# The last stage's first product as Strassen's seven block products, and its second product in a pass of its own

## What is computed

```python
def _moe2_ref(x, w_in, w_out, alpha):          # x: 4608 x 512, w_in: 512 x 2048, w_out: 2048 x 512
    h = x @ w_in
    g = np.maximum(h, 0.0) + alpha * np.minimum(h, 0.0)
    return g @ w_out
```

## Time and profile before

| | |
|---|---|
| time, median of 3 | 1443.22 us (1442.37 to 1443.36) |
| the profiled execution's own time | 1444.12 us |
| its span | 1442.4 us |
| mean granted clock of TensorE | 0.983 |
| busy: PE, DVE, ACT, POOL | 95%, 46%, 28%, 13% |
| chain that ended last, by engine | PE 86%, DVE 5%, ACT 3%, DMA 2% |
| last stage, first matmul to the end of the span | 676.7 to 1442.4 us |

### The profile page before, as it was taken

One profiled execution on the slowest core, in us unless ns is written; L12 is line 12 of the kernel. 1 busy time (PEld: TensorE's weight loads), 2 busy tenths in 40 slices (PEclk: granted clock), 3 DMA queues, 4 the chain that ended last, 5 costly groups with the idle time before them and its releaser, 6 DMA issues.

```text
span 1442.4 us, 18986 instructions
## 1 busy us (share of the span) xinstructions
PE 1366.5 (95%) x6741; PEld 1119.5 (78%) x6742; DVE 659.0 (46%) x949; ACT 398.8 (28%) x632; POOL 189.2 (13%) x234
## 2 busy tenths in 40 slices
PE   4998589999979999996999999999999999999998
PEld 3877468888868888885787878878788787887887
DVE  3677652222545525435545344453544435444343
ACT  5888231112333313223212121121211212112121
POOL 4564121111212212221000000000000000000000
PEclk9999799999989999998999999999999999999999
DMA  7785252111444314133201010010100101001000
GB/s 268 263 272 182 74 192 85 44 44 44 155 141 163 132 71 160 56 141 109 74 0 58 0 49 9 0 58 0 55 3 0 58 0 58 0 4 55 0 30 15
DMA packets 71483, 112.58 MB, mean 78 GB/s; under 512 B 6816, under 2 KB 38560, under 8 KB 70816
## 3 DMA queue, kind: packets, MB, share of 16 engines
q1 hardware_dynamic: 64192, 91.79, 18.8%
q0 software_dynamic: 6112, 19.93, 4.0%
q10 hardware_dynamic: 1152, 0.52, 0.2%
HBM read 84.17 MB, written 27.53 MB: 77 GB/s over the span
## 4 chain that ended last, share of the span: by engine, by line
PE 86%; DVE 5%; ACT 3%; DMA 2%; issue 2%; SPq 2%; DVEq 0%; ACTq 0%; POOL 0%; POOLq 0%
PE ps L320 9%; PE ps L322 9%; PE ps L321 9%; PE ps_o L322 7%; PE ps_o L320 7%; PE ps_o L321 7%; PE ps_y L322 5%; PE ps_y L320 5%; PE ps_h L320 5%; PE ps_y L321 5%; PE ps_h L322 5%; PE ps_h L321 5%; PE ps_hT L1248 2%; SPq L434 2%; PE ps_sr L1139 1%
## 5 line engine op out<-in xcount | busy, mean ns | idle before, releaser
L762 ACT ACTIVATE gT_hi<-act_g 128x512 fp32r<-128x512 f32 (+1 forms) x144 | 87.7, 609 | 563.2 <-DVE act_g L1054 563.2
L1051 DVE TENSOR_SCALAR neg<-ps,alpha 128x512 f32<-128x512 f32 (+1 forms) x144 | 103.7, 720 | 291.1 <-PE ps L322 291.1
L320 PE MATMUL ps<-yT_hi,w_hi 128*128 128x512 f32 (+1 forms) x576 | 221.9, 385 | 5.7 <-DVE yT_lo L1041 5.7
L322 PE MATMUL ps<-yT_hi,w_lo 128*128 128x512 f32 (+1 forms) x576 | 221.0, 384 | 0.0
L321 PE MATMUL ps<-yT_lo,w_hi 128*128 128x512 f32 (+1 forms) x576 | 221.0, 384 | 0.0
L320 PE MATMUL ps_o<-w_hi,gT_hi 128*128 128x512 f32 x544 | 212.0, 390 | 0.9 <-DVE w_lo L793 0.9
L322 PE MATMUL ps_o<-w_hi,gT_lo 128*128 128x512 f32 x544 | 212.2, 390 | 0.0
L321 PE MATMUL ps_o<-w_lo,gT_hi 128*128 128x512 f32 x544 | 211.8, 389 | 0.0
L1057 DVE TENSOR_TENSOR gT_lo<-act_g,gT_hi 128x512 fp32r<-128x512 f32 (+1 forms) x144 | 95.4, 663 | 97.2 <-ACT gT_hi L762 97.2
L320 PEld LDWEIGHTS ps<-yT_hi,w_hi 128*128 128x128 f32 x576 | 108.5, 188 | 32.4 <-DVE yT_lo L1041 9.3
L320 PE MATMUL ps_h<-w_hi,xgT_hi 128*128 128x512 f32 x296 | 122.1, 412 | 9.6 <-DVE w_lo L793 7.7
(11 more groups left out here) (190 smaller groups left out, 1738.0 us busy)
## 6 DMA issues: line engine op xcount, KB each, us to landing
stage<-in_moe_w SPq DMA_DIRECT2D x32, 1024.0 KB
xs_all<-in_xT SPq DMA_DIRECT2D x8, 1024.0 KB, 6.3
xN_all<-in_xN SPq DMA_DIRECT2D x8, 1024.0 KB, 6.2
rows_x<-xrow SPq DMA_DIRECT2D x32, 256.0 KB, 2.5
yg<-rows_y SPq DMA_DIRECT2D x128, 64.0 KB, 1.9
out_rows<-orow SPq DMA_DIRECT2D x32, 256.0 KB, 2.1
stage<-in_moe_w_in SPq DMA_DIRECT2D x4, 1024.0 KB
stage<-in_moe_w_out SPq DMA_DIRECT2D x4, 1024.0 KB
```

The costliest lines, as they stand in the source:

```text
L320: pe.matmul(out, s_hi, m_hi, start=start, stop=False)
L322: return pe.matmul(out, s_lo, m_hi, start=False, stop=stop)
L762: act.activation(gT_hi[:, c % 2, f, 0:w], act_g[:, 0:w], ACT.Copy).then_inc(g_hi_ready, 1)
L1051: dve.tensor_scalar(neg[:, 0:w], ps_1[f][:, 0:w], 0.0, alpha[:, ft:ft + 1], ALU.min, ALU.mult)\
```

## The change

The first product of a batch of 544 rows (512 tokens and 32 state rows, which were a ninth group before) is now Strassen's scheme in Winograd's form. The batch's transposed rows are cut in four blocks (two halves of the 512 inputs by two halves of 272 rows), w_in in four (inputs by features); seven products P1 to P7 of sums of such blocks, each 2x3 matmuls of 272 columns for each of 8 tiles c of 128 features (`product`), take the place of eight. Four sums of w_in's blocks are made on DVE during experts 0, 2, 4 and 6, a quarter of the columns each, from an extra load, stored in memory (`sums_w`), and loaded back; seven chunks of 1 MB follow expert 7 in place of four (`block_of`). Four sums of the rows' blocks are made on DVE, and seven high and seven low parts in place of four, the low ones between c=7's additions. The seven products of a c lie in seven PSUM banks; one ACT copy and seven DVE additions (`add`) put the four quarters of the features together in `gb`, and SP stores them, not rectified, to `acts` in memory. PE waits before each product until the addition that frees its bank is done.

The second product runs after all first products, tile by tile (`down`): SP loads a tile's 16x128 features for 128 rows (1 MB in 512-byte rows; the two tiles of state rows in 128-byte pieces), DVE rectifies in two operations over 2048 elements, ACT and DVE split, PE takes 48 matmuls of 512 columns. Buffers are double. w_out is loaded over `stage` early in the first pass and split during the last batch, in w_in's freed places. At the stage's start the rows of batch 0 are fetched by SP and ACT in half each, and ACT rounds and DVE rests three more weight chunks ahead of them.

The core of the diff:

```diff
-FC = 2
-NC_ = KFF // FC
+NP = KFF // 2
+FH = FF // 2
+TB = S + NS
+TH = TB // 2
+P1, P2, P6, P7, P4, P5, P3 = range(7)
+SLOT = (0, 1, 4, 2, 3, 5, 6)
...
+        tT = yz_[:].rearrange("p (m k t) -> p m k t", m=4, k=2)
+        b_of = (yT[:, 0:2, 0:TH], yT[:, 2:4, 0:TH], tT[:, 1], tT[:, 2], tT[:, 3], tT[:, 0], yT[:, 2:4, TH:TB])
...
+            with sp.Fori(1, E // 2) as pair:
+                load_raw(pair - 1)
+                for par in range(2):
+                    e = 2 * pair + par
+                    for i in range(CH):
+                        load_weights(e * CH + i, i, expert_chunk(e, i), (e - 1) * CH + i + 1)
+                    if par == 0:
+                        store_sums(pair - 1)
+            load_raw(3)
+            block_of = (WI[:, 0:2, 0:FH], WI[:, 2:4, 0:FH], sums_w[2], WI[:, 2:4, FH:FF], sums_w[1], sums_w[0], sums_w[3])
+            for i in range(7):
+                if i == 2:
+                    store_sums(3)
+                load_weights(E * CH + i, i % CH, block_of[i], (E - 1) * CH + i + 1)
...
+            def load_acts(t, g, k, again):
+
+                if again:
+                    wait_apart(sp, g_lo_ready, t - 1)
+                sp.dma_start(gt[k % 2][:], acts[bass.ds(g, 1)].rearrange("a p f t -> (a p) f t")[:, :, k * P:(k + 1) * P])\
+                  .then_inc(g_loaded[k % 2], 16)
+
+            def load_states(t, k):
+                wait_apart(sp, g_lo_ready, t - 1)
+                for j in range(4):
+                    sp.dma_start(gt[k][:, :, j * NS:(j + 1) * NS], acts[4 * k + j][:, :, S:TB]).then_inc(g_loaded[k], 16)
...
+            with sp.Fori(0, B - 1) as g:
+                wait_apart(sp, b_lo_ready, 7 * g + 7)
+                for c in range(NP):
+                    if c < QB:
+                        load_y(g + 1, (c,))
+                    store_acts(g, c)
...
+            for c in range(NP):
+                store_acts(B - 1, c)
+            for par in range(2):
+                for h in range(2):
+                    sp.wait_ge(acts_stored[h][par], 16 * (1 + B * NP // 2))
+            sp.wait_ge(product_ready[P3], B * NP)
+            load_acts(1, 0, 1, False)
...
+                    t = 4 * g + k
+                    load_acts(t + 2, g if k < 2 else g + 1, (k + 2) % 4, True)
+                    store_tile(t, k, [g * TB + k * P])
+            for k in range(4):
+                t = XT - 4 + k
+                if k < 2:
+                    load_acts(t + 2, B - 1, k + 2, True)
+                else:
+                    load_states(t + 2, k - 2)
+                store_tile(t, k, [(B - 1) * TB + k * P])
...
+            round_chunk((E + 1) * CH, 0, 0, 1)
...
+            for i in range(1, 3):
+                round_chunk((E + 1) * CH + i, i, i, 1)
...
+            def copy_p1(g, c):
+
+                n = NP * g + c
+                act.wait_ge(product_ready[P1], n + 1)
+                if not (isinstance(n, int) and n == 0):
+                    act.wait_ge(u2_ready, n)
+                act.activation(part[0][:], ps_p[P1][:, 0:TH], ACT.Copy).then_inc(p1_copied, 1)
...
+            def tile_high(t, k):
+                act.wait_ge(g_ready, t + 1)
+                if not (isinstance(t, int) and t < 2):
+                    act.wait_ge(o_ready, t - 1)
+                act.activation(g_hi[k % 2][:], gt[k % 2][:], ACT.Copy).then_inc(g_hi_ready, 1)
...
+                        dve.wait_ge(raw_loaded, 64 * pair + 64)
+                        dve.tensor_tensor(sum_w[:, 0], raw_w[:, 2], raw_w[:, 3], ALU.add).then_inc(s1_made, 1)
+                        dve.tensor_tensor(sum_w[:, 2], raw_w[:, 0], raw_w[:, 2], ALU.subtract)
+                        dve.wait_ge(s1_made, pair + 1)
+                        dve.tensor_tensor(sum_w[:, 1], sum_w[:, 0], raw_w[:, 0], ALU.subtract).then_inc(s2_made, 1)
+                        dve.wait_ge(s2_made, pair + 1)
+                        dve.tensor_tensor(sum_w[:, 3], raw_w[:, 1], sum_w[:, 1], ALU.subtract).then_inc(sums_made, 1)
...
+            for i in range(3):
+                rest_chunk((E + 1) * CH + i, i, i, 1)
...
+            def sums_12(g):
+                dve.wait_ge(yT_ready, 2 * g + 2)
+                dve.tensor_tensor(tT[:, 0], b12, b11, ALU.subtract).then_inc(t_ready, 1)
+                dve.wait_ge(t_ready, 4 * g + 1)
+                dve.tensor_tensor(tT[:, 1], b22, tT[:, 0], ALU.subtract).then_inc(t_ready, 1)
+
+            def sums_34(g):
+                dve.tensor_tensor(tT[:, 2], b22, b12, ALU.subtract).then_inc(t_ready, 1)
+                dve.wait_ge(t_ready, 4 * g + 2)
+                dve.tensor_tensor(tT[:, 3], b21, tT[:, 1], ALU.subtract).then_inc(t_ready, 1)
...
+                    n, par = NP * g + c, c % 2
+                    again = not (isinstance(n, int) and n == 0)
+                    ahead = c == NP - 1 and not last
+                    dve.wait_ge(p1_copied, n + 1)
+                    free_acts(dve, 0, NP // 2 * g + c // 2, par)
+                    add(gb[par][:, 0, 0:TH], P2, n, part[0][:], c11_ready)
+                    if again:
+                        dve.wait_ge(u5_ready, n)
+                    add(part[1][:], P6, n, part[0][:], u2_ready)
+                    if ahead:
+                        low(g + 1, P1)
+                    dve.wait_ge(u2_ready, n + 1)
+                    if again:
+                        dve.wait_ge(c22_ready, n)
+                    add(part[2][:], P7, n, part[1][:], u3_ready)
+                    if ahead:
+                        low(g + 1, P2)
+                    dve.wait_ge(u3_ready, n + 1)
+                    free_acts(dve, 1, NP // 2 * g + c // 2, par)
+                    add(gb[par][:, 1, 0:TH], P4, n, part[2][:], c21_ready)
+                    if ahead:
+                        low(g + 1, P6)
+                    add(gb[par][:, 1, TH:TB], P5, n, part[2][:], c22_ready)
+                    if ahead:
+                        low(g + 1, P7)
+                        low(g + 1, P4)
+                    add(gb[par][:, 0, TH:TB], P5, n, part[1][:], u5_ready)
+                    if ahead:
+                        low(g + 1, P5)
+                        low(g + 1, P3)
+                    dve.wait_ge(u5_ready, n + 1)
+                    add(gb[par][:, 0, TH:TB], P3, n, gb[par][:, 0, TH:TB], c12_ready)
+                    if not last:
+                        if c == 4:
+                            turn_y(g + 1, 0, 9)
+                        if c == 5:
+                            turn_y(g + 1, 9, 17)
+                            sums_12(g + 1)
+                        if c == 6:
+                            sums_34(g + 1)
+                    else:
+                        for i, f in enumerate((c, NP + c)):
+                            dve.wait_ge(wo_hi_ready, 2 * c + i + 1)
+                            dve.wait_ge(product_ready[P4], n + 1)
+                            dve.tensor_tensor(w_out(w_lo, f), raw_out(f), w_out(w_hi, f).bitcast(F32), ALU.subtract)                               .then_inc(wo_lo_ready, 1)
+                        if c == 5:
+                            rectify(0, 0, 1)
+                        if c == 6:
+                            tile_low(0, 0)
...
+            free = {P1: p1_copied, P2: c11_ready, P6: u2_ready, P7: u3_ready, P4: c21_ready, P5: u5_ready, P3: c12_ready}
+
+            def product(p, g, c):
+
+                n = NP * g + c
+                if c == 0:
+                    pe.wait_ge(b_lo_ready, 7 * g + p + 1)
+                if isinstance(n, int) and n == 0:
+                    pe.wait_ge(w_lo_ready, E * CH + SLOT[p] + 1)
+                else:
+                    pe.wait_ge(free[p], n)
+                for k in range(2):
+                    mm = three(pe, ps_p[p][:, 0:TH], w_in(w_hi, p, k, c), w_in(w_lo, p, k, c),
+                               b_hi[p][:, k, :], b_lo[p][:, k, :], k == 0, k == 1)
+                mm.then_inc(product_ready[p], 1)
+
+            def group(g):
+                for c in range(NP):
+                    for p in range(7):
+                        product(p, g, c)
...
+            def down(t, k, fresh=False):
+                pe.wait_ge(g_lo_ready, t + 1)
+                pe.wait_ge(o_copied, t + 1)
+                for i in range(KFF):
+                    f = i // 2 + i % 2 * NP
+                    if fresh:
+                        pe.wait_ge(wo_lo_ready, i + 1)
+                    mm = three(pe, ps_o[k % 2][:], g_hi[k % 2][:, f, :], g_lo[k % 2][:, f, :], w_out(w_hi, f), w_out(w_lo, f),
+                               i == 0, i == KFF - 1)
+                mm.then_inc(o_ready, 1)
 
             pe.wait_ge(w_lo_ready, CH * (E + 1))
             pe.wait_ge(yT_ready, 1)
             for _ in range(11):
                 pe.matmul(ps_o[0][:], w_hi[0][:, 0:P], w_hi[0][:, 0:DM], start=True, stop=True)
-            with pe.Fori(0, B - 1) as g:
-                group(g, 4)
-            group(B - 1, 4)
-            group(B, 2)
+            group(0)
+            with pe.Fori(1, B) as g:
```

(25 more changed lines are left out.)

349 lines of the change are left out of this document (185 added, 164 removed).

## The result

The changed kernel takes 1427.31 us (median of 4 runs, 1426.94 to 1427.9), the kernel before 1442.86 beside it: ratio 0.9893, 95% interval 0.9875 to 0.991. It is 15.6 us faster, where 11.8 were forecast; 1431.4 was the forecast, 1416 to 1452 the range.

The account below looks back on a forecast made before the run. The last stage was taken as bound by TensorE's matmul columns. 338.7 + 1.6 + 2 + 15.2 + 369.5 + 5 = 732.0 against 760.9 us, with +17.1 at the start: -11.8, so 1431.4 us, range 1416 to 1452.

Parts of the forecast that it names:

- First product: First pass of the last stage: 2688 matmuls of 272 columns at 0.126 us, 338.7 us, a gain of 41.3 us.
- rival d: First product: weight load not hidden at the short width, 0.188 us a matmul, +166 us, 1598; chance 0.02.
- rival (c): First product's short matmuls run at the second product's pace per column, 0.1203 us: -15 us, 1416; chance 0.05.
- Second pass: Second product in its own pass: the same 1632 matmuls at 0.2264 us, 369.5 us, with loads hidden.
- The start: Start of last stage: seven weight blocks in place of four move first product from 676.70 to 693.8, +17.1 us.
- half clock: PE's slow stretch after waiting: 1.6 us charged at the first products, and 1.6 us again after the gap between passes.
- Hand-overs: Batch to batch in the first pass: no stall by a hair, 0.3 us charged for each of 7, 2 us.
- Rival (a): VectorE bounds the hand-overs at c=7 of each batch: 2.9 us each, +18 us, 1450; chance 0.12.
- State tiles: Last two tiles of the second pass, loaded in 128-byte pieces: 5 us of stall.
- rival b: State tiles' loads cost by packet count instead of bytes: +15 us, 1446; chance 0.13.
- Between the passes: Waits of 2.6 us before tile 0 and 11.1 before tile 1, then half clock 1.6: 15.2 us (12 to 20).

Follow-up runs that it names:

- the run with extra work: Changed kernel plus four more unread VectorE subtractions of 224 elements in each of seven batch hand-overs, ahead of P3's last addition: 1434.73 us.
- moved weights: Changed kernel with only allocation order changed, w_hi0 and w_lo0 at 116,128 to 181,664 instead of 17,088 to 82,624: 1415.63 us, ratio 0.9815.

## Why the prediction was right, and where its terms were off

The direction, the time and the main mechanism held: seven products of 272 columns in place of eight of 256, paid for at the start and between the passes. Two of its steps did not: the pace of the second pass, and the cause of the gap before tile 1. 1427.3 lies 4.1 us under the forecast. But that is a sum of errors against each other:

- **First product**, 338.7 forecast at 0.126: measured 0.1257 a step, 338. Right; the weight load of 188 ns stayed hidden (rival d is out), and rival (c)'s 0.1203 is out too.
- **Second pass**, 369.5 at 0.2264: 380.7 at 0.2333, **11.2 us too little, the largest error**. The failed step is "The same 1632 matmuls, in a pass of its own, 369.5 us at 0.2264". I took the duration from the row of the same product. The change put its weights into the low buffer and its features above, which is the pairing of the earlier trace rows, 0.2327. Two rows at 512 columns stood in the trace with 3% between them, and I never asked why they differ. The Trainium skill, TensorE: Matmul & The Clock Gate, section "Wait — 56ns, not 53.3ns?", gives one pace for a width, 0.216 for 512 columns; no run here reaches it, and there are two. Nor did any reach the 0.116 that the forecast worked out from it for 272 columns.
- **The start**, +17.1: from the last yrow to the first product 30.8 us against 17.5, +13.3 (659.24 to 676.70 before, 658.33 to 689.10 after). The links are the forecast's. The sums' store landed at 650.2 and not 651.0; five blocks took 5.6 us each and not 5.9; the last two hardly suffered from the fetch of y (678.40 where I had 683.5, "+3" for the sharing). By the end of the warm-up the clock was nearly up: three matmuls of 0.22 us are left of the half clock at the first products, 0.3 us in place of 1.6.
- **Hand-overs**, 2 us: none, with 0.5 us of slack measured by the run with extra work. Rival (a) did not come, but it was only half a microsecond away.
- **State tiles**, 5 us, or 20 by the count of packets (rival b): none. 1 MB in 128-byte pieces was ready after 9.2 us, where the last such load in 512-byte rows took 6.2 (issued at 1366.92, taken up by VectorE at 1373.10) and the forecast's row 7.1. So neither rate held: 8192 pieces took less than half of the 20.2 us that the count gave, but the small pieces cost some 3 us over the bytes, and the DMA engines were full for it (141 GB/s at a DMA share of 1.11, against 208 GB/s at 0.79 for the load in rows). It was hidden because 9.2 lies under 11.7.
- **Between the passes**, 15.2: 1.8 for the two waits before tile 0, 8.7 before tile 1, 2.6 of half clock, 13 in all. The size was close and the step "Tile 1's features are all stored only after c=7's additions" is wrong: they are batch 0's. SP had the load behind waits for the last stores, and one order changed gave 9.1 us.

Errors: second pass +11.2; start -3.8, its half clock -1.3, hand-overs -2, state tiles -5, between the passes -2, first product -1. In sum -4, as measured. A range that reached 1416 to 1452 held it, but the middle was right by chance to a few microseconds.

What stays open: whether the two paces at 512 columns are parted by a border between 58,048 and 83,360, or by the remainder of the addresses by 64, or by something else that goes with both; and why. Also, in the kernel before, the second product of the last two tiles runs at 0.231 in the middle though both operands lie in the upper class. Its runs of 12 matmuls follow products of 256 columns there, and only near their end do the steps come down to 0.227. The moving operands of both products are in the upper class, so the delay seen above does not cover it, and it was not tried. Lastly, the pass of 272-column products took 340.1 us with moved weights and 340.3 without, so no effect of place shows there; why was not tried either.

## What to carry to other kernels

Where one trace has two paces for the same shape of instruction, find out what separates them before one is used for code that moves: here it was the addresses of the stationary and the moving operand in a partition, 3% of every 512-column matmul. When a run shows that an address matters, list what else changes with the address (its remainder by 32, 64 and 128) before the cause is called a border. When work is split into passes, read the issuing queue at the seam line by line: a load that needs nothing from the stores before it should not stand behind them. And a stage that waits for weights may hide a slower wait behind them, so a repair gives the difference to the next chain, not the whole wait.

## What was not expected of the hardware

- TensorE's step at 512 columns: 0.2265 us with both operands in one of two classes of addresses, 0.2333 with one in each. The lower class ends and the upper begins between 58,048 and 83,360 bytes of a partition; its members also differ by 32 bytes in their remainder by 64, and which of the two counts is open. It did not depend on contiguity of the moving columns, on the bank, on a repeated stationary block, or on what DMAs, VectorE and ScalarE did at the time.
- When the moving operand had come over from the other class, the quick pace took some five to eight steps to set in, after a slow kind and after a quick one: the mean over 24 such matmuls was 0.2279. When only the stationary operand had changed, it was there at once.
- 1 MB in 128-byte pieces took 9.2 us with full DMA engines, beside 6.2 for the same in 512-byte rows.
- A scatter of 256 KB by GpSimd's queue landed after 4.0 us with quiet queues and after 7.4 us beside weight blocks of 1 MB.
